# A three-stage kernel on one core: mixing tiles of four 32-token runs, turned by VectorE from block loads of x

## The reference

```python
# 1: a decayed linear attention, 8 heads of 48 channels
state = alpha[:, :, t, :, None] * state + k_t (outer) v_t;   attn[t] = q_t @ state
# 2: x is attn as [batch, 768 tokens, 384 channels]
theta = x @ w_theta
zr, zi = x * cos(theta), x * sin(theta)
y = einsum('ts,bsd->btd', w_tok_r, zr) + einsum('ts,bsd->btd', w_tok_i, zi)
u = x + y
x = u + maximum(u @ w_ch, 0)
# 3: a gated feed-forward part of 1024 channels
h = maximum(x @ w_in, 0)
conv = 3 taps over the tokens of h, per channel
out = (h / (1 + exp(-conv))) @ w_out
```

## Time and profile before

| | |
|---|---|
| time, median of three runs | 532.39 us (531.52 to 533.65) |
| profiled execution, span from first to last instruction | 530.5 us |
| TensorE busy | 522.1 us, 98% |
| VectorE busy | 441.2 us, 83% |
| ScalarE busy | 287.4 us, 54% |
| GpSimd busy | 72.0 us, 14% |
| moved by DMA | 56.93 MB, 107 GB/s in the mean |

### The profile page before, as it was taken

How to read it: one execution, slowest core, us unless ns; L and a number is a source line. 1 busy time by engine, 2 the same in 40 slices (tenths; PEclk the granted TensorE clock), 3 DMA queues, 4 the chain that set the end, 5 groups by cost and what they waited for, 6 DMA issues and landing times.

```text
span 530.5 us, 11806 instructions
## 1 busy us (share of the span) xinstructions
PE 522.1 (98%) x4142; PEld 513.2 (97%) x4142; DVE 441.2 (83%) x801; ACT 287.4 (54%) x607; POOL 72.0 (14%) x65
## 2 busy tenths in 40 slices
PE   8999999999999999999999999999999999999997
PEld 7999988999999999999999999999999999999997
DVE  8999996997886759767786777999888888889874
ACT  4889887765534434444344542555555454545353
POOL 5988893000000000000000000000000000000000
PEclk9999999999999999999999999999999999999999
DMA  8999987476131020211062011202020110201011
GB/s 326 336 308 361 313 302 224 120 236 222 40 104 31 17 70 25 96 30 54 15 205 94 1 45 56 80 2 90 0 89 30 59 56 33 89 0 47 0 46 44
DMA packets 37163, 56.93 MB, mean 107 GB/s; under 512 B 3328, under 2 KB 27392, under 8 KB 37120
## 3 DMA queue, kind: packets, MB, share of 16 engines
q1 hardware_dynamic: 34000, 51.65, 29.3%
q10 hardware_dynamic: 3120, 4.72, 2.5%
HBM read 42.20 MB, written 14.16 MB: 106 GB/s over the span
## 4 chain that ended last, share of the span: by engine, by line
PE 92%; SPq 2%; DVE 2%; DMA 2%; issue 1%; ACT 0%; POOL 0%; DVEq 0%; ACTq 0%
PE y_bank L1475 26%; PE y_bank L1534 19%; PE theta_bank L1521 10%; PE x_bank L1521 10%; PE y_bank L1505 7%; PE theta_bank L1462 7%; PE weighed L1372 4%; PE x_sum L1330 3%; PE x_sum L1345 2%; PE turned L1357 2%; SPq L734 1%; PE x_bank L1450 1%; DMA x_in<-x_scratch 1%; PE turned L1377 1%; PE x_sum L1316 1%
## 5 line engine op out<-in xcount | busy, mean ns | idle before, releaser
L1534 PE MATMUL y_bank<-first_w,z 128*128 128x384 f32 x576 | 109.5, 335 | 0.0
L1534 PEld LDWEIGHTS y_bank<-first_w,z 128*128 128x128 f32 x576 | 101.2, 188 | 0.0
L1475 PE MATMUL y_bank<-first_w,z 128*128 128x384 f32 x432 | 78.0, 337 | 0.1
L1475 PE MATMUL y_bank<-rest_w,z 128*128 128x384 f32 x432 | 76.9, 336 | 0.0
L1475 PEld LDWEIGHTS y_bank<-first_w,z 128*128 128x128 f32 x432 | 74.5, 188 | 0.3 <-issue 0.3
L1475 PEld LDWEIGHTS y_bank<-rest_w,z 128*128 128x128 f32 x432 | 74.7, 188 | 0.0
L1045 ACT ACTIVATE out_rows<-theta_bank 128x386 f32<-128x386 f32 x32 | 15.8, 493 | 50.6 <-PE theta_bank L1521 50.5
L1275 DVE TENSOR_SCALAR x_rows<-out_rows,taps 128x384 f32<-128x384 f32 x64 | 26.8, 419 | 19.5 <-ACT out_rows L1045 19.4
L1462 PE MATMUL theta_bank<-theta_w,x_t 128*128 128x384 f32 x216 | 41.6, 336 | 0.1
L1278 DVE SCALAR_TENSOR_TENSOR x_rows<-out_rows,taps,x_rows 128x384 f32<-128x384 f32 x64 | 39.6, 619 | 2.3
L1282 DVE SCALAR_TENSOR_TENSOR z_full<-out_rows,taps,x_rows 128x384 f32<-128x384 f32 x64 | 39.6, 619 | 2.2
(11 more groups left out here) (126 smaller groups left out, 974.9 us busy)
## 6 DMA issues: line engine op xcount, KB each, us to landing
a_in<-in_a_rows SPq DMA_DIRECT2D x15, 390.0 KB, 5.8
k_in<-in_k_rows SPq DMA_DIRECT2D x15, 384.0 KB, 5.7
q_in<-in_q_rows SPq DMA_DIRECT2D x14, 384.0 KB, 5.3
v_in<-in_v_tokens SPq DMA_DIRECT2D x16, 288.0 KB, 4.8
x_in<-x_scratch SPq DMA_DIRECT2D x24, 192.0 KB, 2.5
y<-x_all SPq DMA_DIRECT2D x7, 576.0 KB, 3.2
u_scratch<-u_sum ACTq DMA_DIRECT2D x6, 576.0 KB, 3.5
u_first<-u_scratch SPq DMA_DIRECT2D x4, 577.5 KB, 4.4
```

The source lines that it names most:

```text
L1475: ins = pe.matmul(y_bank[2 * d + half][:, 0:HALF], z[s % 2][part][zp][:, d * P:(d + 1) * P], mixing_w(part, wp, s)[:, half_tokens(half)], ...
L1534: ins = pe.matmul(out_bank[half][t][:, 0:MODEL], g[k % 4][gp][:, t * P:(t + 1) * P], out_w[wp][f], start=f == 0 and i == 0, stop=f == FF_T ...
```

## The change

- A mixing tile is no longer 128 tokens in a row. The 768 tokens are four quarters (`GROUPS`) of 192; tile s holds the 32 tokens (`BLOCK`) s*32 to s*32+31 of each quarter. The rows of both token weights are put in that order on the host (`laid_out`).
- x of a batch is kept whole in two tiles, x_even and x_odd (`x_all[b % 2]`), with channels on the partitions, loaded by one DMA per batch (`load(b)`, issued in step 2 of the batch before). `halve`, `lower` and `sums` read it there through a view `x_of(b, s)`; x_in, its three buffers and the copy into x_all are gone.
- The same x is loaded a second time as x_blocks: partition g*32 + i holds, for quarter g, channel n*32 + i of the twelve blocks n. Four DMAs per batch, 32 partitions each (`load_blocks`), issued in step 4 of the batch before, once VectorE has turned that batch's last tile. There is one x_blocks.
- `flip(b, s)` on VectorE makes x_tokens from x_blocks by one transpose instruction that turns twelve 32x32 squares on each quarter of the partitions. `turn` (TensorE) and `hold` (ScalarE) are gone. `flip` of tile s+1 stands first in step s, before the sums in the last step.
- The first batch's x comes in two parts: the tokens of tiles 0 and 1, and the rest (`OPENED`). The first part is three loads with runs of 64 tokens (`load_first(0)`) between weight pieces 0 and 1, and four of blocks (`blocks_first(0)`) behind piece 1. The second part, three and four loads with runs of 128 tokens, is behind pieces 2 and 3 in `pair_tail`.
- All four batches of the mixing are written out; the loop over batches 1 and 2 is gone. The reserve for DMA descriptors made by software is set to 1024 bytes.

```diff
...
+BLOCK = 32
+GROUPS = P // BLOCK
...
             do.load_first(0)
             do.refill_piece(1)
-            do.load_first(1)
-            do.load_first(2)
+            do.blocks_first(0)
...
+        do.load_first(1)
+        do.blocks_first(1)
...
-        do.turn(0, 0)
         do.lower(0, 0)
         do.theta_low()
         do.theta(0, 0)
-        do.turn(0, 1)
         do.scan_state(p)
         do.low(0)
-        do.hold(0, 0)
+        do.flip(0, 0)
         do.high(1)
         do.halve(0, 1)
-        do.hold(0, 1)
...
-            tile(do.load, b, s + 3, last)
+            tile(do.flip, b, s + 1, last)
             if s == T - 1:
                 do.mix(b, s)
                 do.sums(b)
             tile(do.halve, b, s + 2, last)
-            tile(do.hold, b, s + 2, last)
...
             tile(do.sines, b, s + 1, last)
-            tile(do.turn, b, s + 2, last)
...
+            if s == 2 and not last:
+                do.load(b + 1)
             if s == 4 and not last:
                 do.spare(b)
+                do.load_blocks(b + 1)
...
-    mix_batch(0)
-    with eng.Fori(1, LAST, 1) as b:
-        mix_batch(b)
-    mix_batch(LAST, True)
+    for b in range(BATCH):
+        mix_batch(b, b == LAST)
...
+    def x_of(b, s):
+        return x_all[b % 2][:, :, :].rearrange("p a (g t) -> p a g t", g=GROUPS)[:, :, :, s * BLOCK:(s + 1) * BLOCK]
+    OPENING = 2
+    OPENED = slice(0, OPENING * BLOCK), slice(OPENING * BLOCK, SEQ // GROUPS)
+    def by_group(rows):
+        return rows.rearrange("p (g t) -> p g t", g=GROUPS)
+    def grouped(tile):
+        return tile[:, :, :].rearrange("p a (g t) -> p a g t", g=GROUPS)
...
-        def load_tile(b, s):
-            sp.dma_start(x_in[s % 3][:, :, :], x_scratch.rearrange("b (a p) t -> b p a t", p=P)[b, :, :, s * P:(s + 1) * P]
-                         ).then_inc(x_got[s % 3].sem, 16)
-        def load_first(s):
-            if s == 0:
+        def load_first(part):
+            if part == 0:
                 for t in x_stored:
                     t.done(sp, PAIRS_PER_BATCH // 2 - 1)
-            load_tile(0, s)
-        def load(b, s):
-            if isinstance(b, int) and b == 1 and s == 0:
+            for d in range(MODEL_TILES):
+                sp.dma_start(by_group(x_even[:, d, :])[:, :, OPENED[part]],
+                             by_group(x_scratch[0, d * P:(d + 1) * P, :])[:, :, OPENED[part]]).then_inc(opening_x[part], 16)
+        def blocks_first(part):
+            for g in range(GROUPS):
+                sp.dma_start(x_blocks[g * BLOCK:(g + 1) * BLOCK, :, OPENED[part]],
+                             x_scratch.rearrange("b (n p) (g t) -> b g p n t", p=BLOCK, g=GROUPS)[0, g, :, :, OPENED[part]]
+                             ).then_inc(opening_blocks[part], 16)
+        def load(b):
+            if b == 1:
                 x_stored[0].done(sp, 2)
                 all_stored_late(sp, 0)
-            for t in (x_turned, x_low, x_kept):
-                t.before(sp, b * T + s, 3)
-            load_tile(b, s)
+                piece_low.done(sp, SPLIT_EARLY - 1)
+            if b == 2:
                 all_stored_late(sp, 1)
                 all_stored_late(sp, 2)
                 for u, t in enumerate(x_stored):
                     t.done(sp, stored_ahead(PAIRS + u))
+            if b >= 2:
+                u_done.done(sp, b - 2)
+            sp.dma_start(x_all[b % 2][:, :, :], x_scratch.rearrange("b (a p) t -> b p a t", p=P)[b, :, :, :]
+                         ).then_inc(x_got[b % 2].sem, 16)
+        def load_blocks(b):
+            x_flipped.done(sp, b * T - 1)
+            for g in range(GROUPS):
+                sp.dma_start(x_blocks[g * BLOCK:(g + 1) * BLOCK, :, :],
+                             x_scratch.rearrange("b (n p) (g t) -> b g p n t", p=BLOCK, g=GROUPS)[b, g, :, :, :]
+                             ).then_inc(blocks_got.sem, 16)
...
         def halve(b, s):
             n = b * T + s
-            x_got[s % 3].done(act, b * (T // 3) + s // 3)
+            if b == 0:
+                act.wait_ge(opening_x[s >= OPENING], 16 * MODEL_TILES)
+            else:
+                x_got[b % 2].done(act, (b - 1) // 2)
             theta_made.before(act, n, 1)
             x_low.before(act, n, 1)
-            act.activation(x_t[0][:, :, :], x_in[s % 3][:, :, :], ACT.Copy).then_inc(x_high.sem, 1)
-        def hold(b, s):
-            n = b * T + s
-            x_turned.done(act, n)
-            z_done.before(act, n, 2)
-            act.activation(x_tokens[s % 2][:, :], x_bank[:, 0:MODEL], ACT.Copy).then_inc(x_moved.sem, 1)
+            act.activation(grouped(x_t[0]), x_of(b, s), ACT.Copy).then_inc(x_high.sem, 1)
...
+        def flip(b, s):
+            n = b * T + s
+            if b == 0:
+                dve.wait_ge(opening_blocks[s >= OPENING], 16 * GROUPS)
+            else:
+                blocks_got.done(dve, b - 1)
+            z_done.before(dve, n, 2)
+            dve.transpose(x_tokens[s % 2][:, :].rearrange("p (n t) -> p n t", t=BLOCK), x_blocks[:, :, s * BLOCK:(s + 1) * BLOCK]
+                          ).then_inc(x_flipped.sem, 1)
...
-            if s == 0:
-                u_done.before(dve, b, 1)
-            dve.tensor_copy(x_all[:, :, s * P:(s + 1) * P], x_in[s % 3][:, :, :]).then_inc(x_kept.sem, 1)
...
-        def turn(b, s):
-            n = b * T + s
-            x_got[s % 3].done(pe, b * (T // 3) + s // 3)
-            x_moved.before(pe, n, 1)
-            if isinstance(b, int) and b == 0 and s == 0:
-                before_done.done(pe, LAST_PAIR)
-            for d in range(MODEL_TILES):
-                ins = pe.transpose(x_bank[:, d * P:(d + 1) * P], x_in[s % 3][:, d, :], ident[:, :])
-            ins.then_inc(x_turned.sem, 1)
...
-        out[x] = inputs[x].T
+        out[x] = inputs[x].T.reshape(GROUPS, TOKEN_TILES, BLOCK, SEQ).transpose(1, 0, 2, 3).reshape(SEQ, SEQ)
...
```

69 lines of the change are left out of this document (35 added, 34 removed).

## The result

The changed kernel takes 529.88 us (median of 6 runs, 528.24 to 530.35) against 532.3 us of the kernel before in the same comparison: a ratio of 0.9948, 95% interval 0.9931 to 0.9964. That is 2.4 us gained where 6.6 were forecast; 529.88 lies half a microsecond above the range. One run of the kernel before, 571.24 us at a mean granted clock of 0.85, is left out of the comparison that e9, e10 and e11 share. The profiled execution took 529.27, its span is 527.6 (before 530.5).

What follows compares the result with a forecast made beforehand. TensorE's unbroken sequence was taken to bound the kernel, transposes being a link of its chain. The terms -7.26 - 1.10 + 1.6 + 0.1 + 0.1 = -6.56 took 532.39 to 525.8 us, range 524.1 to 529.4.

Steps and rivals of the forecast that it cites:

- Transposes: Mixing tiles on TensorE: 22 of 24 tiles' transposes are on the chain at 0.33 us each, saving 7.26 us.
- The stall: First batch, mixing of tile (0,2): the wait for the late load of x tile (0,4) goes, saving 1.10 us.
- The flip: VectorE's new 128x384 transpose in each mixing tile: about 0.5 us, hidden behind TensorE up to 1.02 us.
- Opening x: Entry to mixing: three loads of 256 B runs delay ScalarE's first rounding by 1.6 us, between 0.6 and 2.0.
- The whole +1.6 lands on the path: Entry: ScalarE's k_tokens eviction and TensorE's `added` of the last pair wait behind the load, so all 1.6 us count.
- Blocks: Next batch's block loads at the first batch's end: landing 9.5 us after issue, of some 12.5 allowed, costing nothing.
- rival C: Batch ends: block loads into 32 partitions at half rate, first batch end loses 1 to 2 us, 527.3; chance 0.07.
- Batch ends: Batch ends: without the turn TensorE waits for VectorE's u_part up to 0.05 us each time, 0.1 in all.
- The marks given: Signs of being wrong: waits for z, u_part or a load in the batches, or first mixing later than 97.6.
- Rival A: Opening: 256 B runs cost double or hold up issues, +3 at first load, 1.7 in first tiles, 528.7; chance 0.12.
- D: Mixing tiles: transposes weren't TensorE's cost, the 0.33 us gap stays and only the stall goes, 533.1; chance 0.05.
- B: Mixing: VectorE's flip sets the pace; 540.6 at 2.3 us a flip, chance 0.07; mild form about 529, chance 0.06.

Runs made afterwards that it cites:

- e9: Changed kernel with four tiles instead of two in the opening x loads, same number of runs, 512 B instead of 256 B each: 531.06 us, ratio 0.9972 of before.
- e10: Changed kernel unaltered, measured and profiled again: 526.22 us, ratio 0.9894 of the kernel before.
- e11: e8 with the second batch's x load moved from step 2 to step 3, behind the weight pieces: 526.76 us, ratio 0.9887 of the kernel before.
- e3: Changed kernel with three unused transposes per mixing tile put back on TensorE at their old places: 534.96 us, ratio 1.0051 of the kernel before.
- e12: Changed kernel unaltered, once more, in a single run: 529.2 us.
- e4: Kernel before, with the change's three opening x loads put ahead of its own first x load, into a spare tile: 538.37 us, ratio 1.0104 of before.
- e2: Changed kernel with 22 dummy matmuls on TensorE ahead of the last pair's `added`: 529.48 us, ratio 0.9948 of the kernel before.
- e7: Changed kernel with 10 dummy matmuls on TensorE ahead of the last pair's `added`: 527.08 us, ratio 0.9899 of the kernel before.
- e1: Changed kernel with opening loads of x and blocks issued before the sync queue's wait for the range decision: 526.36 us, ratio 0.9895 of the kernel before.
- e8: Changed kernel with only the opening x loads issued before the decision, and the first batch's in_rows loaded in step 1: 524.93 us, ratio 0.9877 of before.

## Why the prediction was wrong, point by point

- **What bounds the kernel**: right. Steady mixing is TensorE's chain, and what left it came back in full.
- **Transposes, -7.26**: right. The tile went from 8.13 to 7.80, and e3 brings the 0.33 back.
- **The stall, -1.10**: right. From the first mixing to that of (0,2) are 15.84 us (99.73 to 115.57), exactly 6.48 + 1.56 + 6.24 + 1.56; before they were 17.66. Nothing took its place.
- **The flip, 0.5 and hidden**: right. The group says 572 ns, inside 0.45 to 0.6; VectorE's tile in the first batch is 7.47 us (flips at 116.21 and 123.68), still under 7.80. The estimate of 0.93 from three bf16 transposes, after the Trainium skill, page "VectorE: DVE Perf Modes", section "The three transpose paths", is not borne out for this one instruction of 128x384.
- **Opening x, +1.6 with 2.0 as the bound**: mis-sized. From first issue to x_t are 2.15 more in the profile, up to 2.5 more in e10 and e12 (5.00 against 2.53). The two parts were wrong in opposite ways: the third issue goes out 1.37 after the first, not 0.8 to 0.9, since an issue of 512 runs takes 0.66 and not the 0.47 of a small store; its landing takes 3.29, 0.8 more than before, where the price by packet had nearly 2. The Trainium skill, page "DMA: Bandwidth & Descriptors", section "Specifications", asks for 512 B a run; no run here shows a doubling below it: from e9 to the changed kernel, at the same count, half the bytes landed in 0.6 of the time, and a run of 256 B took 18 ns of an engine where one of 512 B took 29.
- **The whole +1.6 lands on the path**: right as a step, but incomplete, and this is the term that failed. I priced a gap of TensorE at its length. A gap made longer by 2.2 us also cost 1.4 to 1.5 in the matmuls behind it (theta 3.19 against 1.78 in the same kernel), because the granted clock fell. e4 shows the fall in the old kernel, e2 and e7 take it away by filling, e1 and e8 by closing the gap. No row of before could show it, as its clock is 1.00 everywhere; but then the cost of a longer gap was an unknown that should have widened the range upward. The Trainium skill has the rule that I left out: page "TensorE: Matmul & The Clock Gate", section "Part 1: The HAM clock gate", says that an idle array goes back to 1.2 GHz and that activity releases it again. The traces agree in six gaps of eight before `added` (theta at 3.19 for 1.78 in the same kernel), and two gaps there passed without a fall.
- **Blocks "landing 9.5 us after the issue, of some 12.5 allowed", nothing**: wrong, most of all in what was allowed. They landed 10.4 us after the issue, 0.9 later than forecast, and cost 0.7, so only some 9.7 were allowed, not 12.5. VectorE came to the flip 9.2 us after the issue, and from the flip's start to the third u_part are 3.36 us (142.61 to 145.97), with TensorE ready at 145.47; the 3 us or more of slack that I gave the sums weren't there. The load was under-priced besides, and here rival C's mechanism (0.07) is what happened. My 4 us were bytes at about the busiest slice's rate; at 56 ns, 1536 runs are 96 x 56 = 5.4 us, at about 215 GB/s. The 27 ns a packet of the earlier trace rows would have given 2.6, still less. In the later profiles the channel matmuls waited up to 2.5 (e10) and 3.1 us (e7). C's estimate was 1 to 2.
- **Batch ends, 0.05 each**: too small. The channel stage takes 9.65, 9.57 and 9.56 us instead of 9.38, 9.39 and 9.37, 0.2 each.
- **The sum.** The three terms of gain gave 8.4 as forecast. Against them stood 1.8 of costs; measured in the profile are 2.15 (opening), 1.4 (clock), 0.7 (blocks), 0.6 (batch ends), and 0.7 by which the last scan of the attention part started later (76.64, before 75.94). That makes 5.55, and -8.36 + 5.55 = -2.8 against the span's -2.9. The 0.7 I don't count to the change: over all profiles that scan starts between 75.65 and 79.24 us, and the changed kernel has it at 76.36 to 77.26 in three executions.
- **Luck.** The second measurement, 526.22, lies within the range and 0.4 from the forecast. It doesn't bear the sum out: its one profile, of a run of 531.2, has the longer opening (5.00 us to x_t) and a late block load, and of the faster runs nothing is known but their time and their clock of 1.000.
- **The marks given.** The first mixing started at 99.73, beyond the 97.6 named as the point where I would be wrong; waits for u_part over 0.3 us, the other mark, appeared too. Rival A had the right place and a near total (528.7), but its mechanism was not what happened: the issues behind the opening did not make the first tiles wait. D fell with e3, B with the flip's 572 ns.

What stays open: why the clock falls with one gap and not with another of the same length, and what shifts the end of the attention part (in e11 a gap and a fall of the clock there, see above). That the low runs (526.1) had the blocks in time is argued, not shown, as none of them was profiled; that their clock stayed up, the 1.000 of each says. With 45.6 and 381.5 us for the later stretches, their span of 524.3 leaves 97.2 for the first, 0.4 less than the earliest last scan of all profiles and this kernel's shortest entry make (75.65 + 21.96 = 97.6).

## What to carry to other kernels

A wait that TensorE has to sit through may cost more than its length, so at an entry to a stretch of matmuls issue its first loads ahead of unrelated waits on the queue, or fill the gap with work that is known to end in time (both 10 and 22 matmuls kept the clock up here, but 22 outlasted the gap and gave nothing back). When work moves from the bounding engine to one that needs its data in another layout, the new loads become the deadline: price them by runs, target partitions and issue time from rows of like shape, look at how many DMA engines take part, add all that is queued in front, work out what is allowed from when the waiting engine gets there, and put what remains uncertain into the range. And measure such a kernel more than once: the one before had the same median within 0.3 us in four comparisons, the changed one two medians 3.7 us apart, so neither one comparison nor one profile shows its typical loss.
